# Reordering the filling of a fused retention + two-layer MoE kernel: a vector step and two copies ahead of the state update

## The chip, the cores and the metric

One Trainium2 chip, one of its NeuronCores. The metric is the device time of one launch in microseconds (us), taken as the median of several runs. The core's engines are TensorE (PE: matmuls and transposes), VectorE (DVE), ScalarE (ACT), GpSimd (POOL) and SyncE (SP, which here only issues DMAs). Each engine takes its instructions strictly in the order of its own program; they meet through semaphores.

## The reference, cut to what matters

```python
# retention, B=4, H=8, S=768, D=64
for t in range(S):
    state = gamma * state + outer(k[t], v[t])
    y[t] = scale * (q[t] @ state)
x = y as (3072 tokens, 512)
# first block: w_in 512x1024, w_out 1024x512
h = x @ w_in
solu = h * softmax(h)
ln = (solu - mean) / sqrt(var + 1e-6) * g_ln
x = ln @ w_out
# second block: w_in 512x2048, w_out 2048x512
h = x @ w_in
out = (h * cos(h)) @ w_out
```

## The kernel before

**Tiles.** The first half of the kernel works on 24 tiles of 128 tokens (6 per batch, 4 batches). A tile passes through retention in chunk form and the first block; its result y is transposed and stored to a scratch tensor. The second half (from about 450 us on) reads the scratch back in superblocks of 768 tokens and does the second block; it is not touched. All matmuls are done on operands split into a high part (fp32r) and a low part (the float32 value minus the high part): three matmuls in place of one. ScalarE casts the high parts, VectorE and GpSimd subtract for the low parts.

**Steps.** `build` writes one list of steps (name, tile), and `run` (L307) makes each of the four computing engines walk the same list: first `head` (L257 to L272, batch 0, written out by hand where the pipeline fills), then a loop over batches with `body`, then `tail`. For each step an engine emits only its own share, so the place of a step in the list sets its place in each engine's queue. The steps that matter here, for a tile t:

- PK: ACT casts k_h (L786); POOL scales raw q in place (L1012) and subtracts k_l (L1015; the trace shows POOL's subtractions at the helper's line L999).
- PQ: ACT casts q_h (L794, two halves of 64 partitions, after POOL has scaled q); q_l follows, by DVE for tiles 0 and 1 (L1133), by POOL from tile 2 on (two instructions at L999, the second after k_l or v_l of its tile).
- PV: POOL scales raw kn in place (L1021) to "n", and subtracts v_l after ACT's v_h (L789). PN: ACT casts n_h (L799), POOL subtracts n_l (L1044, shown at L999).
- SC: PE multiplies q by k for the scores (12 matmuls); DVE masks them to p_m (L1142), ACT casts p_h (L803). PE's SC waits for k_l and both halves of q_l of its tile and for the state of the tile before (`st_done`). PL0, PL1: DVE's p_l (L1149).
- DL: PE's outer products n by v for the state. ST: DVE adds them to the state s (L1160, L1165). SH: ACT casts s_h (L806) and waits for ST. SL: DVE's s_l (L1168).
- O0, O1: PE's output of retention for two pairs of heads each, ACT's x_h (L812), DVE's x_l (L1175).
- L1a, L1b (in the first tile L1x, L1y, L1b): PE's x by w_in, two halves of 512 columns; DVE's row maximum nmax (L1195) at L1b. L1a of tile t waits for u of tile t-1, which reads the same PSUM banks, and for x_l, one half before its first six matmuls and one before its last six.
- EX: ACT's exp (L830). U: DVE's u = h times e with three short instructions behind it (L1201 to L1210). CEN: DVE's u minus mean (L1215). SQ, VAR: the variance. T0, T1: transposes and z_h, z_l (L1229). L2a, L2b: z by w_out.
- W1H, W1L (u = 0 to 7): ACT's and DVE's high and low part of the weights w_in (u = 0 to 3, L1184) and w_out (u = 4 to 7, L1189, two instructions each). They stand in the head alone.

**SP** doesn't follow the list. It has its own order: inputs of tiles 0 to 2 and the weights first; w_out's loads (L407) wait for W1L of the slot that they overwrite (L400); the inputs of tile t+2 wait for n_l and q_l of tile t (L412, L413).

Of the kernel before, what the change touches and what calls it, by code (L numbers as in the profile page):

```python
# [94 lines left out]
def build(nc, qT, kT, kn, vn, consts, w1_in, w1_out, g_ln, w2_in, w2_out, y_scratch, w2_split,  # L95
          w2o_split, out):
    ctx = ExitStack()
    with ctx:
        def sem(name):
            return ctx.enter_context(nc.semaphore(name))  # L100
# [103 lines left out]
        q_lo = [sem("q_lo_a"), sem("q_lo_b")]  # L204
# [46 lines left out]
        def unit(b, n):  # L251

            offset = n - (TILES - 2)
            inside = n < TILES - 1 and (offset >= 0 or not isinstance(b, int) or b > 0)
            return offset if inside and n >= 0 else None
# [2 lines left out]

        head += [("PK", 0), ("PQ", 0), ("PV", 0), ("PN", 0), ("SC", 0), ("PL0", 0), ("PL1", 0),
# [10 lines left out]
                 ("L2b", 0), ("CEN", 1), ("VAR", 1)]  # L270
        for n in range(4, TILES):
            head += [(name, n - behind) for name, behind in STEP]  # L272
# [15 lines left out]
        def wait(eng, s, batch, tile, per=1, i=0, per_batch=TILES):  # L288


            value = batch * (per_batch * per) + (tile * per + i + 1)
            if not isinstance(value, int):
                assert value.min_val >= 1
                eng.wait_ge(s, value)
            elif value > 0:
                eng.wait_ge(s, value)
# [35 lines left out]
        def heads(x):  # L332

            return x.rearrange("p (h d) -> p h d", h=H)

        def q_by_dve(t, b):

            return isinstance(b, int) and b == 0 and t < FIRST + 1

        def by_dve(t, b):  # L340

            return isinstance(b, int) and b == 0 and t < FIRST

        def q_first(t, b):

            return isinstance(b, int) and b == 0 and t == 2

        def loaded(eng, loads, t, b):

            eng.wait_ge(loads[t % 2], b * (32 * TILES // 2) + 32 * (t // 2 + 1))  # L350

        def unit_wait(eng, s, b, u, per=1):

            wait(eng, s, b, u, per_batch=PER_BATCH, per=per, i=per - 1)
# [640 lines left out]
        def _(pool):  # L995
            pool.memset(mhalf[:, :], -0.5).then_inc(setup, 1)

            def subtract(dst, whole, part):
                return pool.tensor_tensor(dst, whole, part.bitcast(F32), ALU.subtract)  # L999

            def step(name, t, b):
                par = t % 2
                if name == "PK":
                    if by_dve(t, b):
                        return
                    q = raw[:, par, 0, :]
                    loaded(pool, ld_kq, t, b)
                    wait(pool, q_sc, b, t - 1)

                    if not (isinstance(b, int) and b == 0 and t < FIRST + 2):  # L1010
                        wait(pool, pl_done, b, t - 1, 2, 1)
                    pool.tensor_tensor(q, q, qsc, ALU.mult).then_inc(q_sc, 1)  # L1012
                    wait(pool, k_hi, b, t)
                    wait(pool, k_lo, b, t - 1)
                    subtract(k_l[:, par, :], raw[:, par, 1, :], k_h[:, par, :]).then_inc(k_lo, 1)  # L1015
                elif name == "PV":
                    if q_first(t, b) or by_dve(t, b):
                        wait(pool, q_lo[1], b, t)
                    k = heads(raw[:, par, 2, :])
                    loaded(pool, ld_nv, t, b)  # L1020
                    pool.tensor_tensor(k, k, ksc.unsqueeze(2).broadcast_to([128, H, D]),  # L1021
                                       ALU.mult).then_inc(n_sc, 1)
                    if by_dve(t, b):
                        return
                    wait(pool, v_hi, b, t)
                    wait(pool, v_lo, b, t - 1)
                    subtract(v_l[:, par, :], raw[:, par, 3, :], v_h[:, par, :]).then_inc(v_lo, 1)
                elif name == "PQ" and not q_by_dve(t, b):
                    wait(pool, q_hi, b, t)

                    for a in range(2):
                        wait(pool, q_lo[a], b, t - 1)
                        if a == 1:
                            wait(pool, k_lo if q_first(t, b) else v_lo, b, t)
                            wait(pool, q_lo[0], b, t)
                        r = slice(64 * a, 64 * a + 64)
                        subtract(q_l[r, par, :, a, :], raw[r, par, 0, :].rearrange(
                            "p (c t) -> p c t", c=PAIRS), q_h[r, par, :, a, :])\
                            .then_inc(q_lo[a], 1)
                elif name == "PN" and not by_dve(t, b):  # L1040
                    wait(pool, n_hi, b, t)
                    wait(pool, n_lo, b, t - 1)
                    wait(pool, q_lo[1], b, t)
                    subtract(n_l[:, par, :], raw[:, par, 2, :], n_h[:, par, :]).then_inc(n_lo, 1)  # L1044
                elif name == "VAR":

                    wait(pool, var_done, b, t, 2, 1)
                    pool.tensor_tensor(scl[:, par, 2:3], scl[:, par, 1:2], mhalf[:, :], ALU.pow)\
                        .then_inc(scl_done, 1)
                    wait(pool, scl_done, b, t, 2, 0)  # L1050
                    pool.tensor_tensor(scl[:, par, 3:4], scl[:, par, 2:3], rinv[:, par:par + 1],
                                       ALU.mult).then_inc(scl_done, 1)
                elif name == "WS" and unit(b, t) is not None:
                    u = unit(b, t)
                    unit_wait(pool, ld_wi, b, u, 16)
                    unit_wait(pool, wi_lo, b, u - 1)
                    combine(w_raw[:, S1, :], w_raw[:, A21, :], w_raw[:, A22, :], ALU.add)\
                        .then_inc(s1_done, 1)
                    combine(w_raw[:, S3, :], w_raw[:, A11, :], w_raw[:, A21, :], ALU.subtract)
                    unit_wait(pool, s1_done, b, u)  # L1060
                    combine(w_raw[:, S2, :], w_raw[:, S1, :], w_raw[:, A11, :], ALU.subtract)\
                        .then_inc(s2_done, 1)
                    unit_wait(pool, s2_done, b, u)
                    combine(w_raw[:, S4, :], w_raw[:, A12, :], w_raw[:, S2, :], ALU.subtract)\
                        .then_inc(s4_done, 1)
                elif name == "TA":
                    y_sums(0)
                elif name == "YL" and t == P2:
                    y_sum4(0)

            def combine(dst, a, b, op):
                return pool.tensor_tensor(dst, a, b, op)  # L1072

            def y_sums(i):

                pool.wait_ge(ld_y, i * 16 + 16)
                pool.wait_ge(q_lo[1], NT)
                pool.wait_ge(n_lo, NT)
                combine(t_3, b22, b12, ALU.subtract).then_inc(t3_done, 1)
                block_wait(pool, t3_done, i, 1, 0)  # L1080
                combine(t_1, b12, b11, ALU.subtract).then_inc(t1_done, 1)
                block_wait(pool, t1_done, i, 1, 0)
                combine(t_2, b22, t_1, ALU.subtract).then_inc(t2_done, 1)

            def y_sum4(i):

                block_wait(pool, yl_done, i, 7, P2)
                block_wait(pool, t2_done, i, 1, 0)
                combine(t_4, b21, t_2, ALU.subtract).then_inc(t4_done, 1)

            pool.wait_ge(ld_cst, 16)
            run(pool, step)
            with pool.Fori(1, NS) as i:
                y_sum4(i)
# [346 lines left out]
```

## Time and profile before

| | us |
|---|---|
| median of 3 runs (lowest, highest) | 942.89 (942.80, 943.17) |
| the profiled execution: its own time | 942.63 |
| its span in the profile | 940.8 |
| PE busy | 916.5 (97%) |
| DVE busy | 683.2 (73%) |
| ACT busy | 562.4 (60%) |
| POOL busy | 281.7 (30%) |
| granted TensorE clock, mean | 0.995 of full |

The span runs from the first to the last recorded instruction; 1.8 us of the profiled execution's time lie around it. Busy shares are averages over the whole span. "PEclk" is the clock that TensorE was granted: 1.00 is 2.4 GHz, 0.50 is 1.2 GHz. In the rows a start time is in us from the span's start. Instructions of one engine overlap a little in the records (the next one starts up to 0.1 us before the one ahead ends), so what a step costs its queue is read from start to start.

### The profile page before, as it was taken

Reading aid. Unit: us, or ns where it says so; the run is one execution under the profiler, and the core shown is the slowest. Engines: PE = TensorE matmul, PEld = TensorE weight load, DVE = VectorE, ACT = ScalarE, POOL = GpSimd, SP = SyncE. Lnnn points to the kernel's source line nnn. Section 1 sums busy time; section 2 is a strip of 40 time slices with the busy share of each in tenths; the row PEclk is TensorE's granted clock in tenths of the full one; section 3 lists DMA queues with packets and bytes.
Section 4 is the critical chain, followed back from the end, with each engine's and each line's share of the span. In section 5 each row is a group of like instructions: output and inputs, shape, how many; then the busy total and the mean of one; then the engine's idle time right before and its main releaser. Section 6 shows DMA issues by size and latency. Waiting matters only on the chain.

```text
span 940.8 us, 14624 instructions
## 1 busy us (share of the span) xinstructions
PE 916.5 (97%) x4912; PEld 818.4 (87%) x4912; DVE 683.2 (73%) x1050; ACT 562.4 (60%) x923; POOL 281.7 (30%) x284
## 2 busy tenths in 40 slices
PE   3989999999999999999999999999999999999998
PEld 2868888888888888888999999999999999999997
DVE  8977788878888788867666676566766566756564
ACT  5656666667666676646564666464756466645453
POOL 3566677567675776741000000000000000000000
PEclk9999999999999999999999999999999999999999
DMA  8412455534645346247885345644437443454301
GB/s 283 157 68 96 140 208 174 207 129 146 232 166 180 135 173 218 111 154 250 311 300 170 113 124 164 206 116 119 120 115 250 118 123 111 125 177 125 112 8 67
DMA packets 106520, 148.18 MB, mean 158 GB/s; under 512 B 7408, under 2 KB 77040, under 8 KB 106480
## 3 DMA queue, kind: packets, MB, share of 16 engines
q1 hardware_dynamic: 106480, 147.69, 48.0%
q8 instruction: 20, 0.33, 0.1%
q14 instruction: 20, 0.16, 0.1%
HBM read 112.01 MB, written 35.65 MB: 157 GB/s over the span
## 4 chain that ended last, share of the span: by engine, by line
PE 94%; DVE 3%; issue 1%; DMA 1%; POOL 0%; ACT 0%; SPq 0%; POOLq 0%
PE bank L321 30%; PE bank L324 30%; PE bank L323 30%; PE bank L642 2%; PE bank L588 1%; PE bank L679 1%; DVE w1i_l L1184 0%; DVE p_l L1149 0%; DMA raw<-kT 0%; PE bank L590 0%; DVE x_l L1175 0%; DVE p_m L1142 0%; DVE s_l L1168 0%; DVE w1o_l L1189 0%; DMA out<-o_a 0%
## 5 line engine op out<-in xcount | busy, mean ns | idle before, releaser
L321 PE MATMUL bank<-yc_h,ring 128*128 128x384 f32 x448 | 151.5, 338 | 0.0
L323 PE MATMUL bank<-yc_l,ring 128*128 128x384 f32 x448 | 151.3, 338 | 0.0
L324 PE MATMUL bank<-yc_h,ring 128*128 128x384 f32 x448 | 151.0, 337 | 0.0
L1072 POOL TENSOR_TENSOR y_raw<-y_raw,t 128x768 f32<-128x768 f32 x4 | 7.5, 1862 | 361.1 <-DVE yc_l L1260 361.1
L1278 DVE SCALAR_TENSOR_TENSOR gg<-turns,c 128x768 f32<-128x768 int32 x64 | 61.0, 954 | 63.8 <-ACT turns L883 63.8
L889 ACT ACTIVATE gg<-gg 128x768 f32<-128x768 f32 x64 | 54.1, 846 | 80.2 <-DVE gg L1285 80.1
L883 ACT ACTIVATE turns<-c 128x768 int32<-128x768 f32 x64 | 54.2, 846 | 79.1 <-DVE c L1348 76.6
L321 PEld LDWEIGHTS bank<-yc_h,ring 128*128 128x128 f32 x448 | 84.0, 188 | 8.0 <-issue 0.5
L323 PEld LDWEIGHTS bank<-yc_l,ring 128*128 128x128 f32 x448 | 84.2, 188 | 7.2
L321 PE MATMUL bank<-w1i_h,x_h 128*128 128x512 f32 x192 | 78.2, 407 | 9.0 <-DVE x_l L1175 4.0
L324 PEld LDWEIGHTS bank<-yc_h,ring 128*128 128x128 f32 x448 | 84.0, 188 | 0.0
L321 PE MATMUL bank<-w1o_h,z_h 128*128 128x512 f32 x192 | 76.9, 401 | 0.5 <-DVE w1o_l L1189 0.5
L324 PE MATMUL bank<-w1i_h,x_l 128*128 128x512 f32 x192 | 76.0, 396 | 0.0
L324 PE MATMUL bank<-w1o_h,z_l 128*128 128x512 f32 x192 | 75.4, 393 | 0.0
L323 PE MATMUL bank<-w1i_l,x_h 128*128 128x512 f32 x192 | 75.3, 392 | 0.0
L323 PE MATMUL bank<-w1o_l,z_h 128*128 128x512 f32 x192 | 75.0, 391 | 0.0
L324 PE MATMUL bank<-w2o,glo_l 128*128 128x512 f32 x192 | 75.0, 391 | 0.0
L323 PE MATMUL bank<-w2o,glo_h 128*128 128x512 f32 x192 | 75.0, 391 | 0.0
L323 PE MATMUL bank<-w2o,ghi_h 128*128 128x512 f32 x192 | 74.9, 390 | 0.0
L324 PE MATMUL bank<-w2o,ghi_l 128*128 128x512 f32 x192 | 74.8, 390 | 0.0
L321 PE MATMUL bank<-w2o,glo_h 128*128 128x512 f32 x192 | 74.6, 389 | 0.0
L321 PE MATMUL bank<-w2o,ghi_h 128*128 128x512 f32 x192 | 74.6, 388 | 0.0
(130 smaller groups left out, 2405.8 us busy)
## 6 DMA issues: line engine op xcount, KB each, us to landing
ring<-w_split SPq DMA_DIRECT2D x224, 256.0 KB, 2.8
w_split<-w_out SPq DMA_DIRECT2D x16, 896.0 KB, 6.2
w2o_split<-wo_out SPq DMA_DIRECT2D x16, 512.0 KB, 2.9
w2o<-w2o_split SPq DMA_DIRECT2D x8, 1024.0 KB, 7.6
raw<-qT SPq DMA_DIRECT2D x24, 256.0 KB, 2.9
raw<-kT SPq DMA_DIRECT2D x24, 256.0 KB, 2.6
raw<-kn SPq DMA_DIRECT2D x24, 256.0 KB, 3.7
raw<-vn SPq DMA_DIRECT2D x24, 256.0 KB, 4.5
```

The source lines that it names most:

```text
L321: eng.matmul(dst, ah, bh, start=first and i == 0, stop=False, skip_group_check=read_between)
L323: eng.matmul(dst, ah, bl, start=False, stop=False, skip_group_check=read_between)
L324: m = eng.matmul(dst, al, bh, start=False, stop=last_one and i == n - 1, skip_group_check=read_between)
L588: pe.matmul(ps_d[:, p, :, :], n_h[:, par, cols], v_hl[:, :, par, cols], start=True, stop=False)
L642: m = pe.transpose(ps_t[:, k * 128:(k + 1) * 128], c_b[:, (4 * g + k) * 128:(4 * g + k + 1) * 128], ident[:, :])
L679: m = pe.transpose(ps_t[:, k * 128:(k + 1) * 128], y32[:, k * 128:(k + 1) * 128], ident[:, :])
L883: act.activation(turns[:, r, :], flat(c_32[:, r, :, :]), ACT.Copy, scale=INV_2PI)\
L889: act.activation(gg[:, r, :], gg[:, r, :], ACT.Sin, scale=0.5)\
L1072: return pool.tensor_tensor(dst, a, b, op)
L1278: dve.scalar_tensor_tensor(gg[:, r, :], turns[:, r, :], -TWO_PI_HI, flat(c_32[:, r, :, :]), ALU.mult, ALU.add)\
```

## The change

The list `head` gets another order in two places, and one wait of GpSimd is left out for one tile. PK, PQ of tile 2 and W1H of unit 4 move ahead of SC of tile 1. U of tile 1 and O0, L2a, O1 stand ahead of ST and SH of tile 2, which were ahead of O0 and U before; PK to PN of tile 3, which stood ahead of O1, now stand behind it. PN's wait for the second half of q_l is left out for a tile whose q_l is made by VectorE (tile 1).

```diff
-                 ("DL", 0), ("ST", 0), ("W1H", 1), ("W1L", 1), ("PQ", 1), ("L1x", 0), ("PN", 1), ("W1H", 2),
-                 ("W1H", 3), ("W1L", 2), ("SC", 1), ("W1L", 3), ("L1y", 0), ("PK", 2),
-                 ("PQ", 2), ("PL0", 1), ("PL1", 1), ("SH", 0), ("SL", 0), ("W1H", 4), ("L1b", 0),
+                 ("DL", 0), ("ST", 0), ("W1H", 1), ("W1L", 1), ("PQ", 1), ("L1x", 0), ("PN", 1),
+                 ("W1H", 2), ("W1H", 3), ("W1L", 2), ("PK", 2), ("PQ", 2), ("W1H", 4), ("SC", 1),
+                 ("W1L", 3), ("L1y", 0), ("PL0", 1), ("PL1", 1), ("SH", 0), ("SL", 0), ("L1b", 0),
                  ("DL", 1), ("EX", 0), ("ST", 1), ("U", 0), ("O0", 1), ("O1", 1), ("SH", 1),
                  ("PV", 2), ("CEN", 0), ("SQ", 0), ("PN", 2), ("SC", 2), ("SL", 1), ("L1a", 1),
                  ("W1H", 5), ("W1L", 4), ("PL0", 2), ("T0", 0), ("PL1", 2), ("W1L", 5),
                  ("W1H", 6), ("L1b", 1), ("DL", 2), ("T1", 0), ("VAR", 0), ("W1L", 6), ("W1H", 7),
-                 ("W1L", 7), ("EX", 1), ("ST", 2), ("O0", 2), ("SH", 2), ("U", 1), ("PK", 3),
-                 ("PV", 3), ("PQ", 3), ("PN", 3), ("L2a", 0), ("O1", 2), ("SL", 2), ("SQ", 1),
+                 ("W1L", 7), ("EX", 1), ("U", 1), ("O0", 2), ("L2a", 0), ("O1", 2), ("ST", 2),
+                 ("SH", 2), ("PK", 3), ("PV", 3), ("PQ", 3), ("PN", 3), ("SL", 2), ("SQ", 1),
                  ("L2b", 0), ("CEN", 1), ("VAR", 1)]
...
                 elif name == "PN" and not by_dve(t, b):
                     wait(pool, n_hi, b, t)
                     wait(pool, n_lo, b, t - 1)
-                    wait(pool, q_lo[1], b, t)
+                    if not q_by_dve(t, b):
+                        wait(pool, q_lo[1], b, t)
                     subtract(n_l[:, par, :], raw[:, par, 2, :], n_h[:, par, :]).then_inc(n_lo, 1)
```

## Rows read from the trace of the kernel before

**Rows 1.** The page: busy us (share of the span) and instructions of each engine.

```profile
PE 916.5 (97%) x4912; PEld 818.4 (87%) x4912; DVE 683.2 (73%) x1050; ACT 562.4 (60%) x923; POOL 281.7 (30%) x284
```

**Rows 2.** Windows: stretch and length, busy by engine, PEclk, DMA share, GB/s.

```profile
9.38:64.28 54.90, 43.21 (x224) 36.02 (x225) 47.84 (x76) 35.05 (x62) 31.25 (x24) 0.91 0.40 142
64.28:940.80 876.52, 873.31 (x4690) 782.36 (x4688) 628.39 (x962) 523.56 (x856) 250.15 (x255) 1.00 0.48 157
22.40:26.20 3.80, 3.80 (x14) 3.19 (x15) 3.12 (x4) 0.00 (x0) 2.39 (x2) 0.50 0.42 144
60.40:63.80 3.40, 3.40 (x14) 2.94 (x13) 2.33 (x5) 1.48 (x3) 3.23 (x3) 0.50 0.02 5
```

**Rows 3.** Timeline of PE: start, us, instruction, idle before and its releaser.

```profile
23.86 0.55 PE L321 MATMUL bank<-q_h,k_h 128*128 128x256 f32 x1
28.51 0.50 PE L321 MATMUL bank<-w1i_h,x_h 128*128 128x512 f32 x1 [1.22 <-DVE w1i_l L1184]
56.02 0.50 PE L321 MATMUL bank<-w1i_h,x_h 128*128 128x512 f32 x1 [1.63 <-DVE work L1201]
59.82 0.50 PE L321 MATMUL bank<-w1i_h,x_h 128*128 128x512 f32 x1 [2.15 <-DVE x_l L1175]
62.07 0.41 PE L321 MATMUL bank<-q_h,k_h 128*128 128x256 f32 x1
64.28 0.60 PE L642 MATMUL bank<-ident,work 128*128 128x128 f32 x4
```

**Rows 4.** Timeline of ACT and POOL: from s_h of tile 2 to q_l of tile 3.

```profile
53.96 0.62 ACT L806 CAST s_h<-s 128x512 fp32r<-128x512 f32 x1 [4.58 <-DVE s L1165]
...
55.18 1.28 POOL L999 TENSOR_TENSOR k_l<-raw,k_h 128x512 fp32r<-128x512 f32 x1 [3.55 <-ACT k_h L786]
...
60.08 1.56 POOL L999 TENSOR_TENSOR q_l<-raw,q_h 64x512 fp32r<-64x512 f32 x1 [0.17 <-POOL q_l L999]
```

**Rows 5.** Timeline of DVE, the state of tile 2, x_l, and U of tile 1.

```profile
52.09 1.11 DVE L1160 SCALAR_TENSOR_TENSOR s<-s,cst,bank 128x128 f32<-128x128 f32 x4
53.24 0.69 DVE L1165 TENSOR_TENSOR s<-s,bank 128x512 f32<-128x512 f32 x1
53.84 0.85 DVE L1175 TENSOR_TENSOR x_l<-bank,x_h 64x256 fp32r<-64x256 f32 x2
54.73 1.23 DVE L1201 SCALAR_TENSOR_TENSOR work<-bank,work 128x1024 f32<-128x1024 f32 x1
...
56.06 0.16 DVE L1210 RECIPROCAL rinv<-esum 128x1 f32<-128x1 f32 x1
```

**Rows 6.** Timeline: VectorE and GpSimd side by side, 14 to 33 us.

```profile
14.27 1.29 POOL L999 TENSOR_TENSOR k_l<-raw,k_h 128x512 fp32r<-128x512 f32 x1 [1.28 <-ACT k_h L786]
14.31 1.80 DVE L1126 TENSOR_TENSOR n_l<-raw,n_h 128x512 fp32r<-128x512 f32 x1
...
28.38 2.39 DVE L1149 TENSOR_TENSOR p_l<-p_m,p_h 128x512 fp32r<-128x512 f32 x2
30.69 1.77 DVE L1168 TENSOR_TENSOR s_l<-s,s_h 128x512 fp32r<-128x512 f32 x1
32.39 1.21 DVE L1195 TENSOR_REDUCE nmax<-bank 128x1 f32<-128x1024 f32 x1
```

**Rows 7.** Timeline of ACT, DVE and POOL around SC of tile 1.

```profile
19.32 0.62 ACT L799 CAST n_h<-raw 128x512 fp32r<-128x512 f32 x1
...
21.11 1.22 DVE L1184 TENSOR_TENSOR w1i_l<-w_raw,w1i_h 128x1024 fp32r<-128x1024 f32 x1
22.25 1.40 DVE L1133 TENSOR_TENSOR q_l<-raw,q_h 64x512 fp32r<-64x512 f32 x2
...
25.99 1.30 POOL L1012 TENSOR_TENSOR raw<-raw,cst 128x512 f32<-128x512 f32 x1
```

**Rows 8.** DMA issues of single stretches (9.65 to 10.2; 18 to 19): KB, us to landing.

```profile
raw<-qT SPq DMA_DIRECT2D x1, 256.0 KB, 8.4
...
w_raw<-w_out SPq DMA_DIRECT2D x1, 512.0 KB, 3.9
```

## The prediction

> **What bounds the kernel now.** I began with the page: TensorE is busy for 97% of the span [rows 1]. A share like that says that little can be won, but not where, so I cut the span in windows next. From 64.28 us to the end TensorE is busy for 873.31 of 876.52 us [rows 2], and the view of its waits names no wait in that stretch at all. Before it, from 9.38 to 64.28 us, it is busy for 43.21 of 54.90 us, while VectorE is busy for 47.84 [rows 2]. The reader is to see two kernels in one: a filling that VectorE paces, and 876 us that TensorE paces without a hole. All of the change lies in the filling, and behind it nothing that TensorE has to do changes. So the question is one number: when does TensorE start the transposes of tile 1, now at 64.28 us [rows 3]? The end moves by as much.
>
> The timeline of TensorE then gives its last holes. It waits 1.63 us ahead of 56.02 for U of tile 1 and 2.15 us ahead of 59.82 for tile 2's second x_l [rows 3]; SC of tile 3 follows at 62.07 at half the clock (0.50, that is 1.2 GHz, from 60.40 to 63.80 [rows 2]). These two holes are what the second reordering reaches. Behind them stands a third condition that no wait view shows, because it was met just in time: SC of tile 3 also needs q_l of tile 3, and GpSimd ended that at 60.08 + 1.56 = 61.64 [rows 4], 0.43 us before SC began. Whatever removes the two holes alone wins 0.4 us at most. It is this third condition that I follow.
>
> **Part 1, VectorE and GpSimd around SC of tile 1.** First what two rows show. GpSimd's k_l started at 14.27 and VectorE's n_l at 14.31; n_l took 1.80 us, although the second of VectorE's equal instructions needs 0.69 (L1165 [rows 5]), and ended 0.55 us after k_l. At 28.38 two p_l took 2.39 us and s_l took 1.77 [rows 6], with GpSimd's k_l and q_l going on beside them: 4.16 us for three instructions of about 0.6. The two engines take turns, one whole instruction each, where both operands lie in SBUF.
>
> Now the walk. GpSimd's n_l of tile 1 no longer waits for q_l and starts when n_h is there, at 19.32 + 0.62 = 19.94 [rows 7], ending about 21.25 (1.3 us, as the row at 25.99 [rows 7]). W1L of unit 1 starts at 21.11 [rows 7] and loses 0.1: end 22.4. GpSimd's next instructions, which stood behind n_l, are now free too: scaling q of tile 2 (its operand landed at 18.1 us: issued at 9.7, 8.4 to landing [rows 8]), and, because PK of tile 2 now stands ahead of SC in ScalarE's queue, k_l and q_l of tile 2. They meet q_l of tile 1 on VectorE, two instructions that took 1.40 us from 22.25 [rows 7] with GpSimd idle. Taking turns: q scaled 22.35 to 23.65, first q_l to 24.3, k_l to 25.5, second q_l to 26.15. SC of tile 1 waits for that second half: it starts at 26.2, not 23.86 [rows 3], 2.3 us later. TensorE's clock is at half there already [rows 2]; a 256-column matmul then takes 0.213 us from start to start in the timeline, so SC takes 12 x 0.213 = 2.6 us.
>
> No row shows this 64-partition form beside GpSimd, so its price is bounded: 0 if it isn't blocked, 2.5 if it is. I take 2.5, since n_l, p_l and s_l, which differ only in the number of partitions, were all blocked. The page that bears on it: the Trainium skill, "SBUF — State Buffer", section "Who interferes with whom", has a VectorE instruction with two SBUF inputs wait in full for a GpSimd one that reads SBUF, and the other way round. By that rule, with which the rows of n_l, p_l and s_l agree, the term is 2.5; by the lower bound it would be 0.
>
> The delay is passed on: p_m of tile 1 ends at about 29.7, W1L of unit 3 (1.22 us, as unit 1's [rows 7]) at 30.9 instead of 28.46, and TensorE's matmuls with it start at 31.0 instead of 28.51 [rows 3]. In exchange p_l and s_l are free of GpSimd, which has done its work: that saves some 2.3 of the 4.16 us. But nmax stands next in VectorE's queue (32.39 [rows 6]) and needs TensorE's L1b, which ended about then; with L1b 2.4 us later, the saving only makes VectorE wait. From nmax on the queues hold what they held, so part 1 costs **2.4 us** at the end of W1L of unit 7, from 52.1 (ST's start at 52.09 [rows 5]) to 54.5. W1H of unit 4 ahead of SC on ScalarE costs nothing: its weights landed at 22.0 (issued at 18.12, 3.9 to landing [rows 8]) and it ends at 26.3, before p_m at 28.5; without that cover it would be 1.3 us. SP's queue: w_out's loads and tile 3's inputs go out up to 3.6 us later, at 34 at the latest, and are first read after 43 us: nothing.
>
> **Part 2, the state behind U and both x_l.** On VectorE the steps now ahead of ST of tile 2 are U, from 54.73 to 56.06 + 0.16 = 1.49 us; the first x_l, 53.84 to 54.73 = 0.89; the second x_l, of the same shape, another 0.89 [rows 5]. Together 3.27 us. TensorE's O1 of tile 2 stands behind L2a, as before, and its x_h is out by about 56.2, so the second x_l doesn't wait. ST of tile 2 thus ends at 53.93 + 2.4 + 3.27 = 59.6. ScalarE's SH waits for ST, and PK of tile 3 is behind SH in its queue; before, the same SH already waited 4.58 us and released k_h, and GpSimd waited 3.55 us for that k_h [rows 4]. So everything from k_l of tile 3 on moves by 5.67: k_l starts at 60.85, and q_l ends at 61.64 + 5.67 = 67.3. CEN of tile 1 on VectorE met one of GpSimd's instructions before, and meets another now; 0 to 0.5 us more, I take 0.3. SC of tile 3 starts at 67.6.
>
> What it wins: both holes of TensorE go (U is done at 56.0, before TensorE is through with L2b; x_l at 57.8, as its second half is reached), and TensorE is through with L1a of tile 2 at about 60. It then stands idle for about 7.6 us for q_l of tile 3. SC of tile 3 runs wholly at half clock: 2.6 us in place of 64.28 - 62.07 = 2.21 [rows 3].
>
> **The sum.** Start of SC 62.07 to 67.6 is +5.5; SC itself +0.4: the transposes of tile 1 at 70.2, **5.9 us later**. Behind them every engine finds the same distances as before (n_l of tile 3 has 4 us of slack against DL). Span 940.8 + 5.9 = 946.7; with 1.8 around it 948.5; the median of the runs stood 0.26 above the profiled execution: 948.8.
>
> **The rivals.**
> - *VectorE's q_l isn't blocked* (the lower bound of part 1, or other turns than I walked). For it: no row of the form. Then part 2 alone stands: 3.27 - 0.43 + 0.4 = +3.2, 946.1. Chance 0.2.
> - *The clock stays at half beyond SC of tile 3.* Before, it came back during SC of tiles 1 and 3; after an idle 7.6 us it might not: seven of L1b's 512-column matmuls at double their 0.23 us from start to start, +1.6: 950.5. Against: the stretches at half clock end at 26.2 and 63.8, each inside an SC [rows 2]. Chance 0.09.
> - *The savings on p_l and s_l are not lost.* If nmax weren't held by L1b, 2.3 us would come back in VectorE's chain, and with q_l unblocked it would be 3.2 - 2.3 = +0.9: 943.8. Against: nmax started within 0.2 us of L1b's end before. Chance 0.05.
> - *Faster: only the holes count.* If tile 3's k_h and GpSimd's chain didn't hang on SH (were ready by the time that L1a of tile 2 ends), the 1.63 and 2.15 us would go and nothing would follow: 942.9 - 3.8 = 939.1. For it: TensorE's own waits name only these two. Against: GpSimd ended q_l only 0.43 us before SC, and its start hung on ScalarE behind SH [rows 4]. It decides as soon as q_l of tile 3 is there before 62.0. Chance 0.06.
>
> **How the numbers follow.** My forecast has 0.60. A measurement here tells 0.2% (1.9 us) from no change. Forecast, first and second rival are slower by more: 0.89; the third is within: 0.05; faster 0.06. The range takes in the forecast and the first two rivals, with part 1 at its lower bound less half a us, and at the top a third turn of GpSimd (1.3) or the clock: 945.6 to 951.8.
>
> **What would show it.** In the profile after: GpSimd's n_l at about 20 us; VectorE's q_l of tile 1 at two to three times its 1.40 us; SC of tile 1 at 26.2; no hole of TensorE ahead of L1a of tile 2; s of tile 2 done near 59.6 and k_l of tile 3 at 61; one hole of 7 to 8 us ahead of SC of tile 3, released by GpSimd's q_l; transposes of tile 1 near 70. I am wrong if SC of tile 3 starts before 62, or if the stretch behind it shows new waits of TensorE.

## The result, and the profile after

| | before | after |
|---|---|---|
| median (lowest, highest), us | 942.96 (942.80, 943.17), 4 runs | 950.21 (948.92, 952.24), 4 runs |
| profiled execution, its span | 942.63, 940.8 | 952.24, 950.5 |
| start of the transposes of tile 1 | 64.28 [rows 3] | 72.24 |

The change makes the kernel slower: ratio 1.0079, 95% interval 1.0057 to 1.0101. The runs after are spread over 3.3 us (952.24, 948.92, 951.39, 949.03) where those before lie within 0.4 (in the later sets the kernel before spreads over 1.3 to 2.3 us itself, 941.7 to 944.0); the profiled execution is the slowest of them. A second set of five runs of the same kernel gave 949.58, with two runs at 952.1 and 952.3.

Windows of the changed kernel, to be read against [rows 2] (stretch and length; PE, PEld, DVE, ACT, POOL busy; PEclk; DMA share; GB/s):

```profile
9.38:72.24 62.86, 46.26 (x225) 38.98 (x226) 49.55 (x76) 35.35 (x63) 31.51 (x24) 0.84 0.38 124
72.24:950.50 878.26, 874.98 (x4689) 783.56 (x4688) 628.24 (x961) 523.21 (x856) 250.09 (x255) 1.00 0.49 157
72.30:75.60 3.30, 3.30 (x11) 2.77 (x10) 2.55 (x4) 1.35 (x3) 0.00 (x0) 0.51 0.93 312
```

The filling takes 8.0 us more (72.24 against 64.28). The stretch behind it takes 878.26 us against 876.52; TensorE waits for nothing there, but its first 3.3 us run at half clock, which accounts for 1.7. 8.0 and 1.7 are the 9.7 by which the spans differ.

TensorE's waits from 19 to 90 us of the changed kernel (who waited for whom: us in total, times, longest):

```profile
PE bank L321 <- POOL q_l L999: 7.7, 1, 7.7
PE bank L321 <- DVE w1i_l L1185: 4.0, 2, 2.8
PE bank L321 <- POOL k_l L999: 1.9, 1, 1.9
PE bank L321 <- DVE x_l L1176: 1.0, 1, 1.0
PE bank L321 <- DVE w1o_l L1190: 0.5, 1, 0.5
```

The two holes of before, 1.63 for U and 2.15 for x_l [rows 3], are gone. One of 7.7 us stands in their place, ahead of SC of tile 3, and a new one of 1.9 ahead of SC of tile 1. (The profile puts that one down to GpSimd's k_l, which is tile 2's and which SC of tile 1 doesn't wait for; it waits for VectorE's q_l, which ends at 25.87, 0.2 us before SC starts, below. With the wait alone left out, further down, the profile names q_l.)

The first part, in the timeline of DVE, POOL and PE of the changed kernel:

```profile
20.94 1.57 DVE L1185 TENSOR_TENSOR w1i_l<-w_raw,w1i_h 128x1024 fp32r<-128x1024 f32 x1
22.44 3.43 DVE L1134 TENSOR_TENSOR q_l<-raw,q_h 64x512 fp32r<-64x512 f32 x2
25.90 2.18 DVE L1185 TENSOR_TENSOR w1i_l<-w_raw,w1i_h 128x1024 fp32r<-128x1024 f32 x1
29.62 1.80 DVE L1185 TENSOR_TENSOR w1i_l<-w_raw,w1i_h 128x1024 fp32r<-128x1024 f32 x1
36.68 1.23 DVE L1196 TENSOR_REDUCE nmax<-bank 128x1 f32<-128x1024 f32 x1 [3.45 <-PE bank L324]
...
20.16 1.27 POOL L999 TENSOR_TENSOR n_l<-raw,n_h 128x512 fp32r<-128x512 f32 x1 [1.11 <-ACT n_h L799]
21.40 2.25 POOL L1012 TENSOR_TENSOR raw<-raw,cst 128x512 f32<-128x512 f32 x1
23.61 1.71 POOL L999 TENSOR_TENSOR k_l<-raw,k_h 128x512 fp32r<-128x512 f32 x1
29.30 1.04 POOL L1021 TENSOR_TENSOR raw<-raw,cst 128x512 f32<-128x512 f32 x1
...
26.08 0.55 PE L321 MATMUL bank<-q_h,k_h 128*128 128x256 f32 x1 [1.86 <-POOL k_l L999]
```

Reading it: q_l of tile 1 takes 3.43 us, not 1.40 [rows 7], with GpSimd's scaling and k_l inside it, and both of those are stretched too (2.25 and 1.71 against 1.3). SC of tile 1 starts at 26.08, not 23.86. The three W1L that took 1.22 us now take 1.57, 2.18 and 1.80, each meeting an instruction of GpSimd. And at nmax VectorE, which did not wait there before, waits 3.45 us for TensorE; some 1.5 of it is TensorE's clock, which stays at half through most of L1b here (with the first part alone, where L1b ran at full clock, the same wait is 1.98 us).

The second part, DVE, ACT, POOL and PE of the changed kernel, to be read against [rows 4, 5]:

```profile
56.48 1.21 DVE L1202 SCALAR_TENSOR_TENSOR work<-bank,work 128x1024 f32<-128x1024 f32 x1
57.88 1.72 DVE L1176 TENSOR_TENSOR x_l<-bank,x_h 64x256 fp32r<-64x256 f32 x4
60.80 0.69 DVE L1166 TENSOR_TENSOR s<-s,bank 128x512 f32<-128x512 f32 x1
...
61.52 0.62 ACT L806 CAST s_h<-s 128x512 fp32r<-128x512 f32 x1 [3.35 <-DVE s L1166]
...
62.73 1.27 POOL L999 TENSOR_TENSOR k_l<-raw,k_h 128x512 fp32r<-128x512 f32 x1 [6.72 <-ACT k_h L786]
68.07 1.26 POOL L999 TENSOR_TENSOR q_l<-raw,q_h 64x512 fp32r<-64x512 f32 x1 [0.17 <-POOL q_l L999]
...
69.54 0.55 PE L321 MATMUL bank<-q_h,k_h 128*128 128x256 f32 x1 [7.68 <-POOL q_l L999]
72.24 1.05 PE L642 MATMUL bank<-ident,work 128*128 128x128 f32 x4
```

U and x_l first, then the state, then s_h, then GpSimd, which has waited 6.72 us for a k_h that nothing but its place in ScalarE's queue held back; then q_l at 69.33, and SC.

### The profile page after: what moved, and what is told of

Read it like the earlier page. It is cut to its first block, busy times and chain, and to the rows that moved or that the text cites. A ratio compares the mean times of both kernels' runs of the same rounds, so it can differ in the third digit from the quotient of the medians.

```text
span 950.5 us, 14624 instructions
## 1 busy us (share of the span) xinstructions
PE 921.4 (97%) x4912; PEld 822.7 (87%) x4912; DVE 684.7 (72%) x1050; ACT 562.3 (59%) x923; POOL 282.1 (30%) x284
## 4 chain that ended last, share of the span: by engine, by line
PE 93%; DVE 3%; POOL 2%; issue 2%; DMA 0%; ACT 0%; POOLq 0%
PE bank L321 29%; PE bank L324 29%; PE bank L323 29%; PE bank L642 2%; PE bank L588 1%; PE bank L679 1%; POOL raw L1012 1%; PE bank L590 0%; POOL raw L1021 0%; POOL k_l L999 0%; POOL v_hl L999 0%; POOL q_l L999 0%; DVE w1o_l L1190 0%; DMA out<-o_a 0%; DVE p_m L1143 0%
```

## The experiments

Times are medians; each set of runs stands beside runs of the kernel before on the same chip (its median in the table).

| run | us (lowest, highest) | before beside it | ratio (95% interval) |
|---|---|---|---|
| first reordering and wait | 945.43 (944.74, 947.29) | 942.33 | 1.0036 (1.0022, 1.0049) |
| second reordering | 946.89 (946.72, 947.51) | 942.33 | 1.0051 (1.0037, 1.0065) |
| wait alone | 944.53 (942.77, 946.07) | 942.33 | 1.0022 (1.0013, 1.0032) |
| first, GpSimd held back | 943.59 (942.54, 944.41) | 942.33 | 1.0012 (1.0003, 1.0021) |
| second, K of tile 3 early | 939.03 (939.03, 939.60) | 942.71 | 0.9962 (0.9949, 0.9976) |
| change, K of tile 3 early | 943.66 (941.63, 944.06) | 942.71 | 1.0007 (0.9998, 1.0016) |
| change, last hole filled | 948.83 (948.26, 949.74) | 942.71 | 1.0067 (1.0053, 1.0080) |
| second, K and CEN early | 938.74 (938.62, 939.31) | 942.71 | 0.9959 (0.9945, 0.9973) |
| change again | 949.58 (948.98, 952.28) | 942.49 | 1.0088 (1.0074, 1.0103) |
| change, three holes filled | 947.20 (946.83, 949.43) | 942.49 | 1.0056 (1.0042, 1.0070) |
| best order, first hole filled | 940.13 (939.27, 941.28) | 942.49 | 0.9975 (0.9965, 0.9985) |

**The two parts apart.** The first run takes the first hunk of the list and the condition in PN, the second takes the second hunk of the list, both on the kernel before.

> The first reordering and the missing wait alone. My theory (VectorE's q_l of tile 1 takes turns with GpSimd's work for tile 2): q_l of tile 1 about 3.4 us instead of 1.40, SC of tile 1 at 26.1 instead of 23.86, transposes of tile 1 near 66.7 instead of 64.28; 2.4 us longer, 945.4, up to 947 in a run where TensorE's clock stays at half longer. Rival (all the loss is in the second reordering): 943.0. Rival (the saving on p_l and s_l comes through): below 943.

> The second reordering alone. My theory (state of tile 2, then ScalarE's s_h, then k_h of tile 3, then GpSimd's chain, then SC of tile 3): both holes ahead of L1a of tile 2 are gone, s of tile 2 ends at 57.2, k_l of tile 3 starts at 58.4, a hole of 5 to 6 us ahead of SC of tile 3, released by GpSimd's q_l; 3.3 to 3.6 us longer, 946.3. Rival (only TensorE's named holes count): 939 to 940.

Both mechanisms show, each part on its own: 3.1 and 4.6 us over the median beside them, 7.7 together, where the whole change costs 7.1 to 7.3. The sizes were forecast too small (2.4 and 3.3 to 3.6); that the first run met 945.4 so exactly is luck, since the kernel before stood 0.6 us lower in this set. In the first run q_l took 3.43 us again. TensorE in the profiles of the first (one row) and the second run:

```profile
67.17 0.60 PE L642 MATMUL bank<-ident,work 128*128 128x128 f32 x4
```

```profile
65.21 0.55 PE L321 MATMUL bank<-q_h,k_h 128*128 128x256 f32 x1 [7.69 <-POOL q_l L999]
67.91 1.05 PE L642 MATMUL bank<-ident,work 128*128 128x128 f32 x4
```

64.28 became 67.17 with the first part, 2.9 later, and 67.91 with the second, 3.6 later. The first is 0.5 over the 2.4 that I had given it: 0.25 was there at ST already (54.74 against 52.09), and SC of tile 3 itself took 2.52 us where it took 2.21 before, at half clock for longer. The second's hole was 7.7 us, not 5 to 6: TensorE was through with L1a at 57.5, earlier than I had counted, and so waited longer. That changes the hole and not the end. What adds to the end, 0.6 to 0.7 of its 4.6 us, is a clock that stays at half for 1.2 us behind SC. ScalarE's queue shows the chain: it ended O1's x_h at 53.84 and then waited for the state with k_h of tile 3 behind it:

```profile
57.19 0.62 ACT L806 CAST s_h<-s 128x512 fp32r<-128x512 f32 x1 [3.35 <-DVE s L1165]
57.72 0.61 ACT L786 CAST k_h<-raw 128x512 fp32r<-128x512 f32 x1
```

**The wait alone.** Both lists as before:

```diff
-                    wait(pool, q_lo[1], b, t)
+                    if not q_by_dve(t, b):
+                        wait(pool, q_lo[1], b, t)
```

> Only PN's wait is left out for tile 1, both lists as before. By the turns on the port: n_l at about 20, GpSimd scales q of tile 2 from about 22.4, and VectorE's two q_l of tile 1 take 2.6 us (one turn of GpSimd), not 3.4; SC of tile 1 at about 25.0. Time 943 to 944.3, some of the 1.2 us being taken up by later waits. Rival (without a turn: the wait was harmless to leave out): q_l 1.40 us, 943.0 or less.

```profile
22.70 2.47 DVE L1134 TENSOR_TENSOR q_l<-raw,q_h 64x512 fp32r<-64x512 f32 x2
...
25.38 0.55 PE L321 MATMUL bank<-q_h,k_h 128*128 128x256 f32 x1 [0.91 <-DVE q_l L1134]
```

One turn of GpSimd, 2.47 us for q_l, as expected; SC came at 25.38, not 25.0, and the time of 944.53, 2.2 us over before, lies above the 943 to 944.3 expected. The nine runs are spread over 3.3 us, and the clock has a part in it: the four at 945.1 to 946.1 have a mean granted clock of 0.991 to 0.992, the other five 0.994 to 0.995. n_l doesn't read what q_l writes, so the data needed no such wait; but it kept GpSimd out of VectorE's way. Of the first part's 3.1 us, 2.2 thus come with the wait alone; whether the order adds the other 0.9 is within the noise of the two ratios.

**GpSimd held back.** The first part, and in PK of GpSimd for tile 2:

```diff
                     wait(pool, q_sc, b, t - 1)
+                    if q_first(t, b):
+                        wait(pool, q_lo[1], b, t - 1)
```

> As the run with the first reordering alone, but GpSimd waits for VectorE's q_l of tile 1 before it scales q of tile 2, so the two don't meet there; ScalarE's order is that of the change. If the turns are the cause: q_l of tile 1 back to 1.40 us, SC of tile 1 at about 23.9, and most of the 2.4 us is gone: 943.0 to 944. If the order on ScalarE is the cause (p_h of tile 1 behind q_h of tile 2 and W1H of unit 4): as slow as with the first reordering alone, 945.4, or slower, with p_h at 28.7 or later.

```profile
23.20 1.40 DVE L1136 TENSOR_TENSOR q_l<-raw,q_h 64x512 fp32r<-64x512 f32 x2
...
30.17 2.72 DVE L1152 TENSOR_TENSOR p_l<-p_m,p_h 128x512 fp32r<-128x512 f32 x2 [0.67 <-ACT p_h L803]
```

q_l is back at 1.40 us, SC of tile 1 stands behind L1x without a hole (at 24.80, not 23.9), and 1.8 of the 3.1 us are gone, though ScalarE's p_h did come behind q_h and W1H, at 29.54. So the collisions are the greater part of the first part's cost. The 1.3 us that are left are not all explained: p_l waited 0.67 us for that p_h, W1L of unit 1 met GpSimd's n_l (1.57 us), and this execution ran 0.76 us behind that of the first part alone from its first loads on, which can't be held against the edit.

**Is it VectorE's order, or the chain by ScalarE?** Second part, with tile 3's k, v and q ahead of O1, and PN of tile 3 ahead of ST (the fronts of the lines, which are the same, are left out):

```diff
-("O0", 2), ("L2a", 0), ("O1", 2), ("ST", 2),
-("SH", 2), ("PK", 3), ("PV", 3), ("PQ", 3), ("PN", 3), ("SL", 2), ("SQ", 1),
+("O0", 2), ("PK", 3), ("PV", 3), ("PQ", 3), ("L2a", 0),
+("O1", 2), ("PN", 3), ("ST", 2), ("SH", 2), ("SL", 2), ("SQ", 1),
```

> The second reordering alone, but with PK, PV and PQ of tile 3 directly behind the first x_l of tile 2, so that k_h and q_h no longer hang on s_h of tile 2; U and both x_l stay ahead of the state. My theory (it is the chain by ScalarE that makes the second reordering slow, not VectorE's order): k_l of tile 3 starts near 52, its q_l ends near 58.5, the state still ends at 57.2, SC of tile 3 starts at 58.6 and the transposes of tile 1 at 61 to 62; 2.5 to 3.5 us faster than the kernel before. Rival (U and x_l ahead of the state are the cause by themselves): as slow as the second reordering alone, 4 us slower than before.

The profile of this run, ACT, POOL and PE:

```profile
49.41 0.62 ACT L786 CAST k_h<-raw 128x512 fp32r<-128x512 f32 x1
...
51.57 1.75 POOL L999 TENSOR_TENSOR k_l<-raw,k_h 128x512 fp32r<-128x512 f32 x1
56.99 1.28 POOL L999 TENSOR_TENSOR q_l<-raw,q_h 64x512 fp32r<-64x512 f32 x1 [0.17 <-POOL q_l L999]
...
58.48 0.35 PE L321 MATMUL bank<-q_h,k_h 128*128 128x256 f32 x1 [1.04 <-POOL q_l L999]
60.58 0.66 PE L642 MATMUL bank<-ident,work 128*128 128x128 f32 x4 [0.44 <-DVE work L1215]
```

VectorE's order is that of the second part, and the kernel is 3.7 us faster than before and some 8 faster than the second part alone. From 40 to 65 us TensorE's granted clock is full throughout: SC at 58.48 takes 0.36 us for three matmuls. This settles where the second part's cost sits: in SH standing ahead of PK of tile 3, since O1's x_h, the other step ahead of it, was done by 53.84 there.

**The same repair on the whole change.**

> The changed kernel with the same repair: PK, PV, PQ of tile 3 directly behind the first x_l. If the costs of the two parts add and the repair takes away the second one only: 6 to 7 us faster than the changed kernel, and 1 us faster to 1 us slower than the kernel before. Rival (the first reordering needs the second one's order to pay): clearly faster than the second reordering with the repair alone.

943.66, 6.6 us off the change's 950.2 and 4.6 over the run before it. The profiled execution, 941.94, is one of the quick ones: its transposes of tile 1 start at 63.51 against 60.58, 2.9 us later, the same 2.9 as with the first part alone. The eleven runs fall in two groups, four at 941.6 to 942.2 and seven at 943.5 to 944.1; the clock may be a part of it (five of the seven have a mean of 0.993, three of the four 0.994 to 0.995), but two of the seven have 1.000, so the rest stays open. The first part pays in neither order.

**One step further.** CEN of tile 1 also ahead of ST of tile 2 (`("PN", 3), ("CEN", 1), ("ST", 2), ...`):

> As the run with the second reordering and the repair, and CEN of tile 1 also ahead of the state of tile 2, so that the transposes of tile 1 don't wait for it behind s_l. The state ends about 1 us later (58.3), still before GpSimd's q_l of tile 3: SC of tile 3 at 58.6 to 59.3, transposes right behind it at 61; 0.3 to 0.8 us faster than with the repair alone, 3 to 4 us faster than the kernel before. Rival (the transposes didn't wait for CEN): no difference to the repair alone.

938.74, 0.3 us under the repair alone, at the edge of what the runs tell apart (lowest 938.62 and 939.03), and at the low end of the 0.3 to 0.8 expected. The hole of 0.44 ahead of the transposes is gone, the one ahead of SC grew from 1.04 to 1.45, since CEN now meets GpSimd's q_l (the first takes 1.73 us where 1.3 is usual). It is the fastest kernel here: 4.0 us faster than before (0.9959, 0.9945 to 0.9973), 11 faster than the change.

**The clock.** Three runs fill holes of TensorE with matmuls whose result is overwritten, as (here 30 ahead of SC of tile 3):

```diff
+                    if isinstance(b, int) and b == 0 and t == 3:
+                        for _ in range(30):
+                            pe.matmul(ps_t[:, :], w1i_h[:, 0, 0:128], w1i_h[:, 0, 0:512],
+                                      start=True, stop=True)
```

> The changed kernel with 30 matmuls of 512 columns more (6.9 us, their result is overwritten) in TensorE's hole ahead of SC of tile 3. If the half clock behind the hole is what makes the runs scatter between 949 and 952 and part of the cost: SC of tile 3 starts at the same time, at full clock, takes 1.4 us instead of 2.6, and the full clock stays; 1.2 to 4.5 us faster than the changed kernel, 946.5 to 948, with less scatter. Rival (the clock costs only inside SC and the scatter comes from elsewhere): at most 1.2 us, scatter as before. If the 30 matmuls outlast the hole, they cost what they outlast it by.

> The changed kernel once more, unaltered, beside the next run: 949 to 952 as before, in executions of either kind (near 949, near 951.5).

> The changed kernel with TensorE kept busy in three of its holes by matmuls whose result is overwritten: 9 ahead of the second w_in slice of tile 0, 11 ahead of SC of tile 1, 30 ahead of SC of tile 3. If the clock behind the holes is the whole scatter of the changed kernel and some 1.2 us of either part's cost: SC of tile 1 and of tile 3 take 1.4 us each, all runs within 0.5 us of each other, 945.5 to 947.5. Rival (the scatter is not the clock's): runs still 1.5 us or more apart.

The last hole filled: 948.83, and the runs 1.5 us apart instead of 3.3. That is above the 946.5 to 948 expected, and only 0.75 to 1.4 us under the change's two medians, about what the rival allowed; the scatter is what speaks for the clock. Three filled: 947.20, four of five runs within 0.5 us, one at 949.43; the profiled one had the full clock from 19 to 72 us. The change's second set beside it lies at 949.0 to 949.6 and 952.1 to 952.3. Two executions of one and the same program show what the clock does, the profile of the second set (949.58) and the one of the first (952.24):

```profile
29.60:34.50 4.90, 3.66 (x15) 2.50 (x14) 3.64 (x5) 1.14 (x2) 0.76 (x1) 0.90 0.66 200
72.30:75.60 3.30, 3.30 (x21) 2.90 (x20) 2.36 (x4) 0.60 (x2) 1.21 (x1) 1.00 0.89 272
```

```profile
29.60:34.50 4.90, 3.68 (x9) 2.44 (x8) 3.63 (x5) 1.14 (x2) 0.74 (x1) 0.50 0.69 197
```

TensorE in the profile of 949.58, to be read against 69.54 and 72.24 above:

```profile
68.13 0.55 PE L321 MATMUL bank<-q_h,k_h 128*128 128x256 f32 x1 [7.69 <-POOL q_l L999]
70.83 0.95 PE L642 MATMUL bank<-ident,work 128*128 128x128 f32 x4
```

In the slower execution L1b ran at half clock up to 34.6 us and SC of tile 3 came 1.4 us later (69.54 against 68.13); behind it the half clock lasted to 75.6 (the row at 72.30 stands above), in the other it ended at 71.5. The runs without a profile say the same: of the change's nine, the five at 948.9 to 949.6 all have a mean granted clock of 0.991, the one at 951.39 has 0.989, the three at 952.1 to 952.3 have 0.987. So most of this kernel's scatter is TensorE's clock behind holes. It is not so everywhere: the kernel before took 942.3 to 943.0 us in the four executions beside these sets with a mean clock of 1.000, no less than the 941.7 to 942.7 of those at 0.996. The one run at 949.43 with three holes filled has 0.998, as one at 946.83 has, so the clock doesn't explain it, and it stays open.

**Filling the first hole in the best order.**

> The best order so far (repair and early CEN, without the first reordering), and TensorE kept busy by 9 matmuls in its hole ahead of the second w_in slice of tile 0 (from 19.9 to 22.2 us). If the half clock of the kernel before between 19.5 and 26.2 us holds up VectorE through SC of tile 1: SC takes 1.4 us instead of 2.5, the p_m behind it come 1.1 us earlier, and so does everything up to the full stretch: 1 us faster than without, near 937.7. Rival (VectorE's q_l and W1L of unit 2 set the pace there anyway): no difference, 938.7.

A miss on both sides: 1.4 us slower than without, and wider (2.0 against 0.7 us). DVE and PE of this run:

```profile
24.75 1.41 DVE L1146 TENSOR_TENSOR p_m<-bank,cst 128x512 f32<-128x512 f32 x2
26.07 2.12 DVE L1188 TENSOR_TENSOR w1i_l<-w_raw,w1i_h 128x1024 fp32r<-128x1024 f32 x1
28.12 3.46 DVE L1153 TENSOR_TENSOR p_l<-p_m,p_h 128x512 fp32r<-128x512 f32 x2
...
28.25 0.50 PE L321 MATMUL bank<-w1i_h,x_h 128*128 128x512 f32 x1 [2.12 <-DVE w1i_l L1188]
29.20 0.63 PE L321 MATMUL bank<-w1i_h,x_h 128*128 128x512 f32 x1
```

SC of tile 1 took 1.4 us and p_m came 1.2 us earlier, as expected. But GpSimd had started to scale q of tile 2 at 25.85, so W1L of unit 3, which without the filling began at 27.24, just when that was over, now stood behind it and took 2.12 us; p_l went from 2.39 to 3.46. TensorE, early, waited 2.12 us in place of 0.90, and its clock fell behind that hole instead, in the middle of L1b. The turns and the clock both have a part in the loss: the three of the nine runs with a mean clock of 1.000 took 939.3 to 939.6 us, still 0.5 to 0.9 over the run without; the other six, at 0.996 to 0.998, took 940.1 to 941.3.

## Why the prediction was right

The direction, the range (945.6 to 951.8) and both mechanisms held; 948.8 was 1.4 us under the median. Of the terms of the sum, part 1 and the clock were sized too small.

- **"When does TensorE start the transposes of tile 1, the end moves by as much"**: it did, but for the clock: 8.0 of the 9.7 us in the profiled execution, 1.7 behind it.
- **Turns of VectorE and GpSimd.** Forecast for q_l: "two to three times its 1.40", second half at 26.15, SC at 26.2. Measured 3.43 us, 25.87, 26.08. The form that no row had shown is blocked like the others; the lower bound, zero, is out, and with it the first rival, whose 946.1 no run of the change came near. The rule of the Trainium skill ("SBUF — State Buffer", "Who interferes with whom") held, with 3.43 us for 1.40 beside it.
- **"2.4 us at the end of W1L of unit 7"** was mis-sized: in the first part alone ST moved by 2.65 (54.74 against 52.09 [rows 5]), and in the changed kernel's profile at 949.58 U, which stands there, by 2.98 (55.07). The missing term is W1L of unit 3, for which I took 1.22 us and which met GpSimd's scaling of n, at 1.80; in the changed kernel W1L of unit 1 lost 0.35 to GpSimd's n_l as well, where I had counted 0.1.
- **The savings on p_l and s_l** came (1.28 for two p_l in place of 2.39) and were lost at nmax, where VectorE waited: 1.98 us in the first part alone, 3.45 in the slowest execution of the change. The third rival is out.
- **3.27 us for the state, +0.3 for CEN, 7.6 us of hole**: the state moved by 3.2 in the second part alone; the hole was 7.68. CEN cost 0.1 (q_l ended 3.36 us later where k_l started 3.23 later), but SC began 0.2 us after q_l's end (65.21 against 65.00), which the sum took as nothing: that the two together make the 0.3 is luck. The 3.2 us that the first rival left for part 2 alone were 4.3 in its profile; 0.7 of the missing 1.1 is the clock behind SC.
- **The clock** was the second rival, at 0.09, and is what the prediction had too small. I had counted 0.4 us for SC and let the clock come back with SC. In the three profiles that have the second reordering as it was, with no hole filled, it did not: the half clock lasted beyond SC of tile 3 by 1.2 us in the second part alone (0.6 to 0.7 us of time), by 0.7 and 3.3 in the two profiles of the change (0.45 and 1.7, where the rival had named 1.6). In the slower one it also held through most of L1b of tile 0, 1.4 us that no rival had; together about 3. Four of the nine executions of the change, at 951.4 to 952.3, are of that kind or near it. The five steadier ones, at 948.9 to 949.6, are 0.1 to 0.8 over the forecast. In the one of them that was profiled, the transposes of tile 1 start at 70.83, 6.55 us later than before where 5.9 was forecast, which W1L of unit 3 covers; the other 0.45 of its 7.0 us is the clock behind them.
- **"Faster: only the holes count"** is refuted for this change, and half right in its condition: with tile 3's q_l there by 58.3 the kernel did gain, by 3.7 us, as it had named 3.8.

## What to carry to other kernels

When a hole in front of the bounding engine is to be closed, list every condition of the work behind it, also those that were met just in time and which no view of waits shows; here a margin of 0.43 us hid the whole cost. In a list that sets the order of several in-order queues at once, moving a step for one engine moves what stands behind it on all others: ask for each engine what now waits behind the moved step's own wait. And a wait that correctness doesn't need may be what keeps two engines from holding each other up; before it is removed, look at what the freed engine will run next, and beside what.

## What had not been expected of the hardware

- One and the same program gave 949.0 and 952.3 us on one chip. As far as two profiles and the mean clocks of nine runs show it, that is TensorE's clock: where the half clock ended behind a hole differed by 4.0 us between executions, both times (at 30.6 or 34.6; at 71.5 or 75.6). A schedule with holes was here not only longer but less steady; the five runs of the fastest order lay within 0.7 us.
- A full clock is not a gain by itself. With the first hole filled, TensorE handed VectorE its work 1.2 us earlier and the whole became 1.4 us slower.
- VectorE and GpSimd each lose in such a meeting. GpSimd's instructions of 1.3 us took 2.25 and 1.71 us as they waited for VectorE's turn, so a chain on GpSimd is stretched as well.
